# Weights mixed with float32r sums of two numbers in three products, their left-over rows on VectorE and GpSimd, and a reordered last chunk

## The chip, the cores and the metric

The kernel runs on one core of one Trainium2 chip. The metric is the device time of one execution in microseconds, given as the median of several runs.

## What is computed

Two linked computations, all in float32. First an attention through 49 "agent" rows per batch: B = 2, N = 12480 tokens, C = 128 channels. Then a two-layer network (128 to 2048 to 128, a leaky ReLU with a slope of its own for each of the 2048 features) on all 24960 tokens.

```python
a2k = sm(agents, k)            # (2, 49, 12480), softmax over the keys
agent_v = a2k @ v              # (2, 49, 128)
q2a = sm(q, agents)            # (2, 12480, 49)
x = (q2a @ agent_v).reshape(24960, 128)
h = x @ w_in                   # 128 -> 2048
g = np.maximum(h, 0.0) + alpha * np.minimum(h, 0.0)
out = g @ w_out                # 2048 -> 128
```

## The kernel before

x is never made. Since x = P · agent_v, with P the 49 softmax weights of a token, h = P · (agent_v · w_in): the kernel first makes the **mixed weights** M = agent_v · w_in (49 rows by 2048 features) of each batch, and then needs only P. P and M are each carried as two float16 numbers, a high part and what is left over, so that a product has float32's accuracy in three parts. Along the 128 rows of the contraction lie 49 rows of high parts, 49 rows again and the first 30 of 49 (`M_a`, 128 rows by 2048 columns); the remaining 19 rows with a few more (`REST` is 19, kept in groups of 32 rows, four features' tiles below one another) are `M_r`, which holds left-over parts of M.

**M before.** `mix(b, f, bank)` (L594) makes 512 columns of M in a bank of PSUM with one float32 product: `av_m`, the scaled agent values with their columns repeated in the order of the rows of `M_a`, is the stationary side, and `w_in_s[:, f*512:(f+1)*512]` is streamed. ScalarE copies the bank to float16 (`mixed_high`, L1009), VectorE puts the left-over part into rows 96 to 127 where `gate` says so (`mixed_low`, L1246). `mix_rest` (L598, its product in L602) makes the left-over rows by 16 more float32 products of 128 columns with 32 stationary columns each, four side by side in the array; `rest_high` (ScalarE, L1013) and `rest_low` (VectorE, L1251) turn these into `M_r`. `mix_linear` does the same for the linear part of the network. All this happens for batch 0 between the sums over the keys and the first chunk, and for batch 1 in the chunks of the kinds MIX (chunks 20 and 21) and MIX_REST (chunk 22).

**The chunks.** Queries go in 49 chunks: 48 of 512 tokens and a last one (number 48) of 384, half from each batch. A chunk has 8 pairs of feature tiles. For pair p, `tiles(p)` (L650, in the last chunk L647) multiplies `M_a` with the turned softmax weights `PT` into two banks, `rest_of_quad(q)` (L667, L660) adds the left-over rows for two pairs at a time with `M_r`, ScalarE makes `r_hi` (ReLU to float16, L1041), VectorE makes `r_lo` (what is left over, L1296), and `second_layer(p)` (L677) adds three products, in this order: w_hi·r_hi, w_lo·r_hi, w_hi·r_lo, each for two tiles, into the bank `OUT`. Pairs go through three slots of two banks; so `tiles(p)` waits until `r_lo` of the pair three places before it has been read out (`lo_ready`). Scores of the next chunk's queries, and of the second batch's keys in the chunks up to 10, go into the bank `SMALL` between the products of `second_layer` (L618, L868); `mix` for batch 1 uses the same bank, and the next scores wait until it has been read.

**Order around the change.** Every engine's order of work is written out by hand, engine by engine, with semaphores between them. On TensorE for batch 0: `mix(0,0)`, `mix_rest`, `mix_linear`, `tiles(0)`, `tiles(1)`, `rest_of_quad(0)`, `mix(0,1)`, `mix(0,2)`, `mix(0,3)`, and then the body of chunk 0: `second_layer(0)`, second group (`tiles(2)`, `tiles(3)`, `rest_of_quad(1)`), `second_layer(1)`, `tiles(4)`, `tiles(5)`, `rest_of_quad(2)`, `second_layer(2)` and `(3)`, `linear`, `tiles(6)`, `tiles(7)`, and so on. In MIX chunks VectorE's order is `relu_lo(3)`, `mixed_low`, `query_lo`, `relu_lo(4)`, `relu_lo(5)`; the second `mix` of the chunk lies between `second_layer(4)` and `second_layer(5)`. GpSimd has little to do: it adds the two parts of the output (`y`, L462) and copies a few columns of the stack of softmax weights (`query_again`, L443).

**The weights' place.** `w_in_s` (2048 columns, float32) is loaded by one DMA, and VectorE multiplies it by signs (L1343) for each of its four parts of 512 columns. In front of it lie the keys and behind it the values in the queue of SyncE.

## Time and profile before

| | us |
|---|---|
| runs: median (lowest to highest of 3) | 900.53 (900.29 to 901.55) |
| the profiled execution | 901.17 |
| its span from first to last instruction | 899.4 |
| TensorE matmul busy | 892.1 (99%) |
| VectorE busy | 619.2 (69%) |
| ScalarE busy | 502.4 (56%) |
| GpSimd busy | 105.5 (12%) |
| granted TensorE clock | 1.0 of full speed (2.4 GHz) |

A row of the timeline gives the start in us from the start of the span, the time from the first start to the last end of a merged group, the engine, the line, the operation, what it writes and reads by the program's names, and the number of instructions; in brackets the idle time of the engine before it and what released it. TensorE's instructions are pipelined: a group's time contains the end of the last one, so the distance between the starts of two groups is what the first costs. A float32 product is two instructions in the trace, and PEld is the weight load, which overlaps with the stream.

### The profile page before, as it was taken

The page shows a single profiled execution, that of the slowest core. Times are in us where ns is not written, and L with a number is a line of the kernel's source. Part 1 is how long each engine was busy: PE and PEld are TensorE (multiplying, and loading weights), DVE is VectorE, ACT ScalarE, POOL GpSimd, SP SyncE. Part 2 cuts the span into 40 slices and gives each one's busy share as a digit, 9 for nine tenths or more (in the row PEclk, how much of TensorE's full clock was granted, in tenths as well). Part 3 has the DMA queues.
Part 4 walks back from the last instruction along what each step waited for, and adds up shares of the span by engine and source line. Part 5 has one row for each costly group of instructions (what it writes and reads, how often), then busy time and mean ns, then how long its engine had stood idle before and what let it go on. Part 6 is the DMA issues. An engine that isn't in the chain of part 4 may idle for free.

```text
span 899.4 us, 15332 instructions
## 1 busy us (share of the span) xinstructions
PE 892.1 (99%) x5496; PEld 451.9 (50%) x5496; DVE 619.2 (69%) x883; ACT 502.4 (56%) x653; POOL 105.5 (12%) x130
## 2 busy tenths in 40 slices
PE   9999999999999999999999999999999999999998
PEld 9855555555544545444444444444444444444444
DVE  4877767766776667678666676667667676766664
ACT  2445565555555555565555566556565655665554
POOL 6500010001000100010001001011010010010100
PEclk9999999999999999999999999999999999999999
DMA  9952223122322341111112112111111121121110
GB/s 358 359 155 82 62 64 103 58 63 69 98 83 85 98 130 43 39 45 53 36 39 62 35 40 61 35 41 58 38 42 54 39 56 38 39 61 33 30 36 21
DMA packets 69975, 66.13 MB, mean 74 GB/s; under 512 B 36368, under 2 KB 54192, under 8 KB 69552
## 3 DMA queue, kind: packets, MB, share of 16 engines
q1 hardware_dynamic: 69504, 65.45, 23.9%
q8 instruction: 25, 0.41, 0.2%
q10 hardware_dynamic: 432, 0.16, 0.1%
q14 instruction: 14, 0.11, 0.0%
HBM read 41.54 MB, written 12.78 MB: 60 GB/s over the span
## 4 chain that ended last, share of the span: by engine, by line
PE 96%; DMA 2%; DVE 1%; ACT 0%; issue 0%; SPq 0%; DVEq 0%; ACTq 0%
PE ps L677 57%; PE ps L650 18%; PE ps L667 7%; PE ps L618 3%; PE ps L480 2%; PE ps L868 2%; PE ps L565 1%; PE ps L692 1%; DMA kv_s<-vP 1%; DVE r_lo L1296 1%; PE ps L595 1%; PE ps L557 1%; DMA kv_s<-kT 1%; PE ps L703 1%; PE ps L510 0%; ACT r_hi L1041 0%
## 5 line engine op out<-in xcount | busy, mean ns | idle before, releaser
L1296 DVE SCALAR_TENSOR_TENSOR r_lo<-ps,r_hi 128x1024 f16<-128x1024 f32 (+1 forms) x392 | 468.3, 1215 | 247.2 <-ACT r_hi L1041 246.8
L1041 ACT ACTIVATE r_hi<-ps 128x1024 f16<-128x1024 f32 (+1 forms) x392 | 388.6, 1017 | 261.0 <-PE ps L667 254.7
L677 PE MATMUL ps<-r_hi,w_hi 128*128 128x512 f16 (+1 forms) x784 | 244.5, 380 | 0.1
L677 PE MATMUL ps<-r_hi,w_lo 128*128 128x512 f16 (+1 forms) x784 | 241.3, 378 | 0.0
L677 PE MATMUL ps<-r_lo,w_hi 128*128 128x512 f16 (+1 forms) x784 | 234.2, 378 | 0.0
L650 PE MATMUL ps<-PT,M_a 128*128 128x512 f16 x768 | 197.6, 379 | 0.4 <-DVE r_lo L1296 0.3
L462 POOL TENSOR_TENSOR y<-y_relu,y_lin 128x512 f32<-128x512 f32 x48 | 60.7, 1266 | 599.6 <-ACT y_relu L1137 404.1
L677 PEld LDWEIGHTS ps<-r_hi,w_lo 128*128 128x128 f16 x784 | 84.5, 109 | 76.0
L677 PEld LDWEIGHTS ps<-r_lo,w_hi 128*128 128x128 f16 x784 | 78.9, 104 | 78.0
L650 PEld LDWEIGHTS ps<-PT,M_a 128*128 128x128 f16 x768 | 74.7, 98 | 81.3 <-DVE r_lo L1296 2.4
L677 PEld LDWEIGHTS ps<-r_hi,w_hi 128*128 128x128 f16 x784 | 66.7, 104 | 87.3 <-issue 40.0
L667 PE MATMUL ps<-PR,M_r 32*128 32x512 f16 x576 | 75.1, 385 | 0.0
L667 PE MATMUL ps<-PT,M_r 32*128 32x512 f16 x192 | 73.8, 384 | 0.0
L618 PEld LDWEIGHTS ps<-agents,q_s 128*128 128x128 f32 x384 | 66.6, 190 | 10.2 <-issue 0.2
L618 PE MATMUL ps<-agents,q_s 128*128 128x49 f32 x384 | 60.5, 243 | 0.0
L667 PEld LDWEIGHTS ps<-PT,M_r 32*128 32x128 f16 x192 | 17.3, 90 | 81.4 <-issue 81.0
L1033 ACT ACTIVATE stack<-q_p 128x196 f16<-128x196 f32 x49 | 18.3, 373 | 61.1 <-DVE q_p L1287 58.8
L1137 ACT ACTIVATE y_relu<-ps,out_unscale 128x512 f32<-128x512 f32 x48 | 33.0, 687 | 33.8 <-PE ps L677 33.8
L443 POOL TENSOR_TENSOR stack<-stack,ones 128x120 f16<-128x120 f16 x49 | 19.6, 400 | 163.8 <-ACT stack L1033 163.8
L1114 ACT ACTIVATE y_lin<-ps,lin_unscale 128x512 f32<-128x512 f32 x48 | 32.7, 682 | 0.0
L868 PEld LDWEIGHTS ps<-agents,kv_s 128*128 128x128 f32 x176 | 30.8, 191 | 2.6 <-DVE M_a L1246 0.4
L1161 DVE TENSOR_REDUCE k_top<-S 128x49 f32<-128x392 f32 (+2 forms) x26 | 19.9, 775 | 12.2 <-ACT S L997 12.2
(166 smaller groups left out, 491.2 us busy)
## 6 DMA issues: line engine op xcount, KB each, us to landing
q_s<-qT SPq DMA_DIRECT2D x48, 256.0 KB, 2.8
out<-y SPq DMA_DIRECT2D x48, 256.0 KB, 2.1
kv_s<-kT SPq DMA_DIRECT2D x23, 512.0 KB, 4.5
kv_s<-vP SPq DMA_DIRECT2D x12, 512.0 KB, 8.9
kv_s<-vS SPq DMA_DIRECT2D x6, 1024.0 KB, 6.1
PR<-PT SPq DMA_DIRECT2D x147, 32.0 KB, 1.9
PT<-stack SPq DMA_TRANSPOSE x196, 2.4
w_lin<-w_out SPq DMA_DIRECT2D x1, 1024.0 KB, 10.2
```

The lines of the kernel that those rows point to most:

```text
L443: pool.tensor_tensor(stack[0:T, :, 2 * A:128], stack[0:T, :, REST:A], ones[0:T, 0:4 * SPARE].rearrange("p (t a) -> p t a", a=SPARE), ALU.m ...
L462: pool.tensor_tensor(y[:, half, :], y_relu[:, half, :], y_lin[:, half, :], ALU.add).then_inc(y_ready, 1)
L618: return pe.matmul(ps[0:T, SMALL, t * A:(t + 1) * A], q_s[:, half, t * T:(t + 1) * T], agents[:, b * A:(b + 1) * A], start=True, stop=True)
L650: pe.matmul(by_tile(ps[:, 2 * slot(p) + u, 0:CHUNK]), M_a[:, b, f:f + 128], tokens(PT, half), start=True, stop=False)
L667: mm = pe.matmul(by_tile(ps[:, 2 * slot(2 * q + u // 2) + u % 2, 0:CHUNK]), M_r[32 * u:32 * u + 32, b, q * 128:(q + 1) * 128], tokens(src[ ...
L677: mm = pe.matmul(ps[:, OUT, 0:wide], w[:, 2 * p + u, :], r[:, s, u, 0:wide], start=(p == 0 and u == 0 and k == 0), stop=(p == PAIRS - 1 an ...
L868: mm = pe.matmul(ps[:, SMALL, t * A:(t + 1) * A], kv_s[:, half, t * KT:(t + 1) * KT], agents[:, A:2 * A], start=True, stop=True)
L1041: act.activation(r_hi[:, p % RING, :, 0:wide], ps[:, at:at + 2, 0:wide], ACT.Relu).then_inc(hi_ready, 1)
L1114: act.activation(y_lin[:, half, :].rearrange("p (h n) -> p h n", n=HALF), ps[:, 2 * LIN_SLOT:2 * LIN_SLOT + 2, 0:HALF], ACT.Copy, scale=li ...
L1137: act.activation(y_relu[:, half, :], ps[:, OUT, 0:CHUNK], ACT.Copy, scale=out_unscale[:, b, :]).then_inc(relu_saved, 1)
L1161: dve.tensor_reduce(k_top[:, b, m, :], by_agent(piece(b, m)), AX.X, ALU.max).then_inc(k_maxed, 1)
L1296: dve.scalar_tensor_tensor(out=r_lo[:, p % RING, :, 0:wide], in0=ps[:, at:at + 2, 0:wide], scalar=0.0, in1=r_hi[:, p % RING, :, 0:wide], o ...
```

## The change

`w_in` is split into two float32r numbers, `w_in_hi` (rounded by a ScalarE copy) and `w_in_lo` (a GpSimd subtraction), and so are the scaled agent values, `av_hi` and `av_lo` (two more VectorE steps). `mix` makes three float32r products hi·hi, hi·lo, lo·hi instead of one float32 product. `mix_rest`, `rest_high` and `rest_low` are gone: the left-over rows are taken from the same bank as `M_a`'s, by four subtractions of 19 rows by 128 columns for each `f`, written to four groups of 32 rows. VectorE does them for `f` = 0 of batch 0 and all four of batch 1 (`mixed_rest`); GpSimd does `f` = 1, 2, 3 of batch 0 (`mixed_rows`) from a float32 copy in SBUF that ScalarE makes (`mixed_out`), together with the work of `mixed_low` for them. For batch 0 the second `mix` is moved to the place of `mix_rest`. `w_in` is loaded in two DMAs into `y_lin` and `y_relu`, `w_inT` into `r_lo`, which are free until the first chunk. In the last three chunks the first two products of `second_layer(4)` go before `tiles(7)`, and in the last chunk `second_layer(7)` begins with its four products of `r_hi` before `r_lo` is there. `M_r` is cleared by GpSimd at the start.

```diff
             def mix(b, f, bank):
-                pe.matmul(ps[:, bank, :], av_m[:, b, 0:128], w_in_s[:, f * 512:(f + 1) * 512], start=True,
-                          stop=True).then_inc(m_raw, 1)
-
-
-            def mix_rest(b, bank):
-                for t in range(FT):
-                    q, g = t // 4, t % 4 * 32
-                    mm = pe.matmul(ps[g:g + 32, bank, q * 128:(q + 1) * 128], av_m[:, b, 128:SEL],
-                                   w_in_s[:, t * 128:(t + 1) * 128], start=True, stop=True, skip_group_check=True)
-                mm.then_inc(r_raw, 1)
+                pe.wait_ge(win_lo, f + 1)
+                at = slice(f * 512, (f + 1) * 512)
+                pe.matmul(ps[:, bank, :], av_hi[:, b, :], w_in_hi[:, at], start=True, stop=False)
+                pe.matmul(ps[:, bank, :], av_hi[:, b, :], w_in_lo[:, at], start=False, stop=False)
+                pe.matmul(ps[:, bank, :], av_lo[:, b, :], w_in_hi[:, at], start=False, stop=True).then_inc(m_raw, 1)
...
             pe.wait_ge(b_av, 1)
             mix(0, 0, F_BANK[0])
-            mix_rest(0, REST_BANK[0])
+
+            pe.wait_ge(b_rows, 2)
+            mix(0, 1, F_BANK[1])
             mix_linear(0, LIN_BANK[0])

             pe.wait_ge(k_saved, FULL + 1 + EARLY)
-            pe.wait_ge(m_low, 1)
+            pe.wait_ge(m_first, 1)
             pe.wait_ge(q_turned, 64)
             tiles(0, 0, 0)
             tiles(1, 0, 0)
-            pe.wait_ge(r_low, 1)
+            pe.wait_ge(r_first, 1)
             pe.wait_ge(q_spread, 48)
             rest_of_quad(0, 0, 0)
-            mix(0, 1, F_BANK[1])
-            pe.wait_ge(l_low, 1)
+
             mix(0, 2, F_BANK[2])
...
                     if start:
 
-                        second_layer(0, half, wide)
-                        pe.wait_ge(m_low, 3)
+                        second_layer(0, half, wide, None, (0, 1))
+                        pe.wait_ge(lo_ready, 1)
+                        second_layer(0, half, wide, None, (2,))
+
+                        pe.wait_ge(m_out, 2)
+                        pe.wait_ge(l_low, 1)
+
+                        pe.wait_ge(m_low, 1)
+                        pe.wait_ge(r_low, 1)
                         second_group()
...
                     pe.wait_ge(lo_ready, g + 2)
+                    if start:
+
+                        pe.wait_ge(m_low, 2)
+                        pe.wait_ge(r_low, 2)
                     tiles(4, half, b)
...
                         elif kind == MIX:
-                            pe.wait_ge(m_low, 5 + 2 * half)
+                            pe.wait_ge(m_second, 1 + 2 * half)
+                            pe.wait_ge(r_second, 1 + 2 * half)
...
+                    if start:
+
+                        pe.wait_ge(m_low, 3)
+                        pe.wait_ge(r_low, 3)
                     tiles(6, half, b)
+
+                    early = 0 if there(n + 3) else 1
+                    second_layer(4, half, wide, None, range(0, early))
                     pe.wait_ge(lo_ready, g + 6)
                     tiles(7, half, b)
                     rest_of_quad(3, half, b)
                     rest_of_linear(half, b)
-                    second_layer(4, half, wide)
+                    second_layer(4, half, wide, None, range(early, 3))
...
                     second_layer(6, half, wide)
-                    pe.wait_ge(lo_ready, g + 8)
-                    second_layer(7, half, wide)
+                    if there(n + 1):
+                        pe.wait_ge(lo_ready, g + 8)
+                        second_layer(7, half, wide)
+                    else:
+
+                        pe.wait_ge(hi_ready, g + 8)
+                        second_layer(7, half, wide, None, (0, 1))
+                        pe.wait_ge(lo_ready, g + 8)
+                        second_layer(7, half, wide, None, (2,))
```

On GpSimd (before `query_again(1)`, and the new rows after it) and on ScalarE and VectorE:

```diff
+            for f in range(FT // 4):
+                at = slice(f * 512, (f + 1) * 512)
+                pool.wait_ge(win_hi, f + 1)
+                pool.tensor_tensor(w_in_lo[:, at], w_in_bank(f), w_in_hi[:, at], ALU.subtract).then_inc(win_lo, 1)
             query_again(1)
+            def mixed_rows(f):
+                pool.wait_ge(m_high, f + 1)
+                pool.wait_ge(m_out, f)
+                m = M_a[96:128, 0, f * 512:(f + 1) * 512]
+                then(pool.tensor_scalar(m, m, gate[96:128, :], None, ALU.mult))
+                pool.tensor_tensor(m, m, mixed_s[96:128, f % 2, :], ALU.add).then_inc(m_low, 1)
+                pool.wait_ge(m_low, f)
+                for u in range(4):
+                    at = f * 512 + u * 128
+                    mr = pool.tensor_tensor(M_r[32 * u:32 * u + REST, 0, f * 128:(f + 1) * 128],
+                                            mixed_s[0:REST, f % 2, u * 128:(u + 1) * 128], M_a[0:REST, 0, at:at + 128],
+                                            ALU.subtract)
+                    if u < 3:
+                        then(mr)
+                mr.then_inc(r_low, 1)
+                pool.wait_ge(r_low, f)
...
             mixed_high(0, 0, F_BANK[0])
-            rest_high(0, REST_BANK[0])
+            mixed_high(0, 1, F_BANK[1])
+            mixed_out(1, F_BANK[1])
             linear_high(0)
             relu_hi(0, 0, 0, True)
-            mixed_high(0, 1, F_BANK[1])
+            relu_hi(1, 0, 1, True)
             mixed_high(0, 2, F_BANK[2])
-            relu_hi(1, 0, 1, True)
+            mixed_out(2, F_BANK[2])
             mixed_high(0, 3, F_BANK[3])
+            mixed_out(3, F_BANK[3])
...
+                then(dve.tensor_scalar(av_m[:, :], av_raw[:, 0:128], m_scale[:, b, 0:1], M_SCALE, ALU.mult, ALU.mult))
+                then(dve.tensor_copy(av_hi[:, b, :], av_m[:, :]))
+                dve.tensor_tensor(av_lo[:, b, :], av_m[:, :], av_hi[:, b, :], ALU.subtract).then_inc(b_av, 1)
...
+            def mixed_rest(b, f, bank):
+                dve.wait_ge(r_clear, 1)
+                dve.wait_ge(m_high, FT // 4 * b + f + 1)
+                for u in range(4):
+                    at = f * 512 + u * 128
+                    mr = dve.tensor_tensor(M_r[32 * u:32 * u + REST, b, f * 128:(f + 1) * 128],
+                                           ps[0:REST, bank, u * 128:(u + 1) * 128], M_a[0:REST, b, at:at + 128], ALU.subtract)
+                mr.then_inc((r_first, r_second)[b], 1)
```

## Rows read from the trace of the kernel before

**Rows 1.** The page: span and busy time by engine.

```profile
span 899.4 us, 15332 instructions
PE 892.1 (99%) x5496; PEld 451.9 (50%) x5496; DVE 619.2 (69%) x883; ACT 502.4 (56%) x653; POOL 105.5 (12%) x130
```

**Rows 2.** Busy time by stretch: length, PE, PEld, DVE, ACT, POOL, clock, DMA.

```profile
46.00:50.00 4.00, 3.21 (x49) 2.51 (x49) 1.68 (x3) 0.00 (x0) 0.00 (x0) 1.00 1.01 263
...
54.70:58.60 3.90, 3.90 (x51) 2.00 (x50) 2.85 (x8) 1.62 (x4) 0.00 (x0) 1.00 0.76 249
```

**Rows 3.** Timeline of TensorE, the mixing for batch 0 and chunk 0.

```profile
54.70 1.09 PE L595 MATMUL ps<-w_in_s,av_m 128*128 128x512 f32 x2
55.72 1.08 PE L602 MATMUL ps<-w_in_s,av_m 128*32 128x128 f32 x32
...
58.59 2.84 PE L595 MATMUL ps<-w_in_s,av_m 128*128 128x512 f32 x6
61.27 0.59 PE L677 MATMUL ps<-r_hi,w_hi 128*128 128x512 f16 x2
...
62.57 1.03 PE L650 MATMUL ps<-PT,M_a 128*128 128x512 f16 x4
...
65.93 1.03 PE L650 MATMUL ps<-PT,M_a 128*128 128x512 f16 x4
```

**Rows 4.** Timeline of VectorE and ScalarE in the same stretch.

```profile
54.04 0.30 DVE L1236 TENSOR_SCALAR av_m<-av_raw,m_scale 128x160 f32<-128x160 f32 x1
...
55.82 0.60 ACT L1009 ACTIVATE M_a<-ps 128x512 f16<-128x512 f32 x1 [1.28 <-PE ps L595]
...
56.45 0.76 DVE L1246 SCALAR_TENSOR_TENSOR M_a<-M_a,gate,ps 32x512 f16<-32x512 f16 x1 [0.53 <-ACT M_a L1009]
...
58.71 1.02 ACT L1041 ACTIVATE r_hi<-ps 128x1024 f16<-128x1024 f32 x1 [0.82 <-PE ps L667]
```

**Rows 5.** Groups by line, of GpSimd and VectorE: busy us, mean ns, idle before.

```profile
L462 POOL TENSOR_TENSOR y<-y_relu,y_lin 128x512 f32<-128x512 f32 x48 | 60.7, 1266 | 599.6 <-ACT y_relu L1137 404.1 <-issue 195.6
L443 POOL TENSOR_TENSOR stack<-stack,ones 128x120 f16<-128x120 f16 x49 | 19.6, 400 | 163.8 <-ACT stack L1033 163.8
L422 POOL TENSOR_SCALAR sigma<-sigma 128x16 f32<-128x16 f32 x1 | 0.3, 283 | 0.1
...
L1257 DVE TENSOR_TENSOR L_b<-ps,L_rh 64x128 f16<-64x128 f32 x2 | 0.6, 282 | 0.0
```

**Rows 6.** Timeline of VectorE, one operation beside GpSimd's work and without it.

```profile
36.65 0.86 DVE L1287 TENSOR_TENSOR q_p<-q_e,q_rec 128x196 f32<-128x196 f32 x1
...
45.33 0.36 DVE L1287 TENSOR_TENSOR q_p<-q_e,q_rec 128x196 f32<-128x196 f32 x1
```

**Rows 7.** Timeline of TensorE and VectorE in chunk 20 (MIX) and chunk 22.

```profile
424.22 0.76 DVE L1246 SCALAR_TENSOR_TENSOR M_a<-M_a,gate,ps 32x512 f16<-32x512 f16 x1
...
425.58 2.35 DVE L1296 SCALAR_TENSOR_TENSOR r_lo<-ps,r_hi 128x1024 f16<-128x1024 f32 x2 [0.22 <-ACT r_hi L1041]
...
427.85 1.03 PE L650 MATMUL ps<-PT,M_a 128*128 128x512 f16 x4
...
456.16 1.08 PE L602 MATMUL ps<-w_in_s,av_m 128*32 128x128 f32 x32
457.18 0.61 PE L677 MATMUL ps<-r_hi,w_hi 128*128 128x512 f16 x2
```

**Rows 8.** Timeline of chunks 47 and 48, the last two.

```profile
876.44 0.59 PE L650 MATMUL ps<-PT,M_a 128*128 128x512 f16 x2
877.21 0.60 PE L650 MATMUL ps<-PT,M_a 128*128 128x512 f16 x2 [0.18 <-DVE r_lo L1296]
...
894.02 0.49 PE L677 MATMUL ps<-r_hi,w_hi 128*128 128x384 f16 x2
...
894.27 0.96 DVE L1296 SCALAR_TENSOR_TENSOR r_lo<-ps,r_hi 128x768 f16<-128x768 f32 x1 [0.37 <-ACT r_hi L1041]
895.29 0.50 PE L677 MATMUL ps<-r_hi,w_hi 128*128 128x384 f16 x2
```

More of the change, by code:

```diff
@@ L112, in build @@
         av_abs = sb("av_abs", [C, A])
-        av_m = sb("av_m", [C, B, SEL])
+        av_m = sb("av_m", [C, 128])
+        av_hi = sb("av_hi", [C, B, 128], F32R)
+        av_lo = sb("av_lo", [C, B, 128], F32R)
         av_l = sb("av_l", [C, B, SEL])
@@ L1412, in body @@
                         mixed_low(1, 2 * half, SMALL)
[L1413 to L1414 removed]
+                        mixed_rest(1, 2 * half, SMALL)
                     if there(n + 2):
```

92 lines of the change are left out of this document (50 added, 42 removed).

## The prediction

> **What bounds the kernel now.** I read the page first: TensorE is busy 99% of the span, and no other engine above 69% [rows 1]. Then the busy time by stretch, to find where TensorE is not full. From 46 to 50 us it is busy 3.21 us of 4.00 with a DMA share of 1.01: the transfers of the values set the pace there [rows 2], so nothing that only moves work of ScalarE, VectorE or GpSimd before 50 us can cost or gain. From 54.7 us on it is full (3.90 of 3.90) [rows 2]. From there on a TensorE instruction that goes is worth its time, and an operation added elsewhere costs nothing until TensorE waits for it. So three places decide: the mixing for batch 0 with chunk 0, the MIX chunks, and the end. Last I read the timeline of these.
>
> **Batch 0: what goes.** The two float32 instructions of the first mix start at 54.70; the next group starts at 55.72. Six instructions (three mixes) start at 58.59 and last 2.84 us [rows 3], of which the last instruction's own tail is about 0.2, so a mix is (2.84 - 0.2)/3 = 0.87 us, or 0.43 for one of its two instructions. No row shows a float32r product. Bounds: as cheap as float16's 512 columns, whose pairs cost (1.03 - 0.16)/4 = 0.22 us each within a group of four [rows 3]; as dear as a whole float32 product, 0.87. I take 0.22, because a float32 instruction of 0.43 is just two streams of 0.22 (so a float32 product is four streams), and I assume that an operand of float32r, having no second part, is streamed once. A mix is then 3 x 0.22 = 0.65, 0.21 less. The trade stops paying at 0.87/3 = 0.29 us a product.
> The Trainium skill (FP8 and Floating Point Precision, TensorE Precision Notes) says the same of float32, four passes, and that the reduced form truncates to 22 bits on reading; by one pass a product the sum stays as it is.
> mix_rest costs 1.02 us in chunk 22, from 456.16 to the start of second_layer at 457.18 [rows 7], and about as much at 55.72.
>
> **Batch 0: what comes instead.** I follow each engine.
> (a) VectorE now makes av_m, av_hi and av_lo in a dependent row. av_m starts at 54.04 and takes 0.30 [rows 4]; two more steps at 0.3 bring b_av to about 54.95, so TensorE starts at 55.05 in place of 54.70: +0.35. Three products end at 55.70, where two float32 instructions ended at 55.55. ScalarE's M_a copy comes 0.27 after the end of the stream (55.82 [rows 4]), now at 55.95; VectorE's 0.76 [rows 4] follow, so tiles(0) starts near 57.4, as before plus 0.1.
> (b) The second mix ends at 56.35. ScalarE: M_a copy to 57.2, the new mixed_out(1), at the 0.60 of the M_a copy [rows 4], to 57.8. linear_high after it is behind nothing that TensorE waits for soon.
> (c) GpSimd's mixed_rows. Its prices: two-input operations of 512 columns 1.27 us and of 120 columns 0.40; a one-input operation of 16 columns 0.28 [rows 5]. The gate multiplication has one input and 512 columns: between 0.28 and 1.27, I take 0.7. The addition: 1.27. Four subtractions of 128 columns: 4 x 0.42 = 1.7. Each waits for the one before, some 0.09 each, 0.5 together. One f is 4.2 us (3.4 to 5.0).
> For the gate multiplication, the Trainium skill (GPSIMD Engine Reference, Engine selection) calls one-input operations "roughly line-rate" and two-input ones about twice as slow as VectorE; by it the estimate is at most 0.65, where I take 0.7 from between the rows.
> So f = 1 is ready at 57.9 + 4.2 = 62.1, f = 2 at 66.4, f = 3 at 70.7.
> (d) TensorE: tiles(0) to rest_of_quad(0) until 58.75, two mixes until 60.05. second_layer(0) has r_hi then (ScalarE's 1.02 us from about 58.9, cf. 58.71 [rows 4]); its last part waits for r_lo until 61.2 and ends at 61.65. The second group waits for bank 4: ScalarE has relu_hi(0), relu_hi(1), the M_a copy and mixed_out(2) in a row from 58.9, 2 x 1.02 + 2 x 0.60, until 62.15. GpSimd's f = 1 comes at 62.1. So the second group starts at 62.25, where it was 62.57 [rows 3]: the TensorE time saved so far has nearly all turned into waiting. second_layer(1) with its scores ends 3.36 us later (65.93 - 62.57 [rows 3]), at 65.6, and there tiles(4) waits for f = 2 until 66.5. It was 65.93: **+0.6**. The f = 3 rows (70.7) are early for tiles(6), some 5.3 us after tiles(4). With 3.4 us an f it would be -0.3, with 5.0 (f = 2 at 67.9) +2.0.
> (e) VectorE beside a busy GpSimd: the same multiplication takes 0.86 us there and 0.36 alone [rows 6]. GpSimd's four subtractions for w_in_lo (4 x 1.27, from about 46.1) end near 51.3, where the scaling of the selection (0.3 us, on the way to av_m) may be held some 0.1. In chunk 0 query_sum and query_norm may be held 1 us, which the 0.6 above covers. **+0.1** (0 to 0.5).
> The skill (GPSIMD Engine Reference, Key points) names contention for VectorE instructions with two SBUF inputs or in a 2-port mode. The 0.86 agrees; relu_lo, with one input in PSUM, should stay as it is.
> Under cover: ScalarE's four roundings of w_in (2.4 us) lie in its wait from 45.5 to 50.1, behind the DMA-bound stretch [rows 2]; the clear of M_r is at GpSimd's idle start; query_again(2) queues behind mixed_rows until 71, and its transposes have their old time at lin_ready, near 73. If that cover went, chunk 2 would wait.
>
> **Batch 1 (MIX).** VectorE gets mixed_rest behind mixed_low: four subtractions of 128 columns from PSUM. The nearest row is 0.28 for that very shape in 64 rows [rows 5]; back to back some of it overlaps, so 0.95 for four (0.6 to 1.15). In chunk 20, mixed_low starts at 424.22 and the next two relu_lo at 425.58 after 0.22 idle, ending at 427.93 [rows 7]. They now end at 427.93 + 0.95 - 0.22 = 428.66. tiles(7) starts 0.43 behind tiles(6), at 428.28 [rows 7], and waits for them: 428.71, +0.43, whatever TensorE saved before. (The wait for r_second before the scores falls into the same loss.) The second mix of the chunk saves its 0.21; its mixed_rest fits into 1.3 us of VectorE's idle time. Two chunks: 2 x (0.43 - 0.21) = **+0.4** (-0.8 without the stall, +0.9).
> MIX_REST: mix_rest gone, nothing in its place, **-1.0**.
>
> **End.** In chunk 47, tiles(6) starts at 876.44 and its two products are over at 876.87; tiles(7) starts at 877.21, released by r_lo [rows 8]. That 0.34 is filled with 0.43 of second_layer(4): -0.34, and the same in chunk 46. In chunk 48 the same gap is filled, but r_lo(6) sets what follows, so nothing is gained there. second_layer(7) starts at 895.29, when r_lo is done (894.27 + 0.96) [rows 8]. second_layer(6) started at 894.02 with 0.98 of products, so the four early ones run from 895.0 to 895.65 and the last two to 895.98 instead of 896.27: -0.3. **-1.0** (-0.3 to -1.1).
>
> **Sum:** +0.6 + 0.1 + 0.4 - 1.0 - 1.0 = -0.9, against the profiled execution's 901.17 (span 899.4 and 1.8 around it), so 900.3. That execution was 0.6 above the median of 900.53. For the median: **899.7 us**. Ends together: -3.3 (897.2) and, with the dear ends of (c), (e) and MIX, +2.2 (902.7).
>
> **Rivals.**
> 1. *No new waits.* GpSimd needs 3.4 us an f or less and VectorE's four subtractions hide. Then each mix's 0.21 counts: start -0.3, MIX -0.85, rest -1.0, end -1.1: 897.3. For it: VectorE is only 69% busy. Against it: VectorE has just 0.22 us of idle time before relu_lo(4) [rows 7]. Halfway cases, one of two stalls gone, reach 898.5.
> 2. *GpSimd is the new bound.* If its step takes 5.5 us, by contention or by slow dispatch of small operations in 32 rows, f = 2 ends at 68.9 and tiles(4) is 3 us late: 899.7 + 2.4 = 902.1. It decides from 3.9 us an f, from which tiles(4) is late at all.
> 3. *float32r isn't cheap.* At 0.43 a product (both halves of a float32 instruction) a mix is 1.29, 0.43 more than before; MIX +1.7, the start about +2.2 since both mixes are ahead of GpSimd's rows, with the -2.0 of rest and end: 902.5, slower. At 0.87 a product: a mix 2.6, MIX +6.8, start +4.5: about 910. It decides from 0.29 us. For it: float32 products pay double per instruction. Against it: the operands have no second part to stream.
> 4. *The end's order does nothing*, because r_lo comes later by as much: 900.7.
>
> **How the numbers follow.** Forecast with rival 4 and the small shifts: 0.66. Rival 1 and its halfway cases: 0.22. Rival 2: 0.05. Rival 3: 0.07. About 0.2% (1.8 us) is what a measurement of this kernel can tell from no change. Below 898.7: rival 1's better part and the low edge of the forecast, 0.22. Above 902.3: rival 3, part of rival 2, and the forecast's edge, 0.12. Within: 0.66. The range takes in the ends of the sum, 897.1 to 902.7, and leaves out the dear case of rival 3.
>
> **What would show it.** L650 of pair 4 near 66.5 with a wait for a GpSimd line before it, mixed_rows of f = 2 ending there; the second group near 62.25; float32r products 0.22 apart; in chunks 20 and 21 a gap of 0.4 us of TensorE ahead of tiles(7) or second_layer(3), released by VectorE; 1.0 us less in chunk 22; no gap after tiles(6) in chunks 46 and 47, and the last product 0.3 us after r_lo plus two products. It is wrong if float32r products are more than 0.29 apart, if GpSimd's step is far from 4.2 us, or if something before 50 us moves the whole.

## The result and the profile after

| | before | after |
|---|---|---|
| median of 7 runs (lowest to highest), us | 900.78 (900.29 to 902.0) | 904.24 (902.34 to 904.74) |
| profiled execution, us | 901.17 | 904.19 |
| span, us | 899.4 | 902.5 |
| mean granted TensorE clock of the span | 1.0 | 0.996 |

The kernel is slower: the ratio is 1.0038, with a 95% interval of 1.0029 to 1.0046. The forecast was 899.7 us and no change that can be measured; the time lies above the upper end of the range, 902.7. In 6 of the 7 runs of the kernel after the mean clock was below 1.0; the seventh, at 1.0, took 902.34 us.

The page of the kernel after, first its busy times, then the clock in 40 slices:

```profile
span 902.5 us, 15292 instructions
PE 892.6 (99%) x5440; PEld 454.2 (50%) x5440; DVE 625.6 (69%) x902; ACT 505.0 (56%) x658; POOL 125.7 (14%) x153
...
PEclk9989999999999999999999999999999999999999
```

TensorE has 56 instructions fewer and yet is busy 892.6 us, where it was 892.1 [rows 1]. One slice of the clock (45 to 68 us) shows an 8. The shares say no more, so I compared positions: in each chunk the addition of y on GpSimd starts at a time that can be read in both traces, and the difference between the kernels tells where the time went.

| chunk | start before, us | after against before, us |
|---|---|---|
| 0 | 80.18 | +4.14 |
| 19 | 419.31 | +4.14 |
| 20 (MIX) | 437.61 | +4.61 |
| 21 (MIX) | 455.90 | +5.09 |
| 22 (MIX_REST) | 474.16 | +4.07 |
| 45 | 853.25 | +4.07 |
| 46 | 869.47 | +3.72 |
| 47 | 885.43 | +3.37 |
| end of the span | 899.4 | +3.1 |

All that is lost is lost ahead of chunk 0's end, and a little in the two MIX chunks; chunks 1 to 19 and 23 to 45 are untouched. The busy times by stretch of the kernel after (length, PE, PEld, DVE, ACT, POOL, clock, DMA share, GB/s) show the kind of the loss, beside [rows 2]:

```profile
50.00:54.70 4.70, 3.35 (x24) 3.08 (x24) 3.72 (x11) 0.72 (x3) 2.38 (x3) 0.90 0.26 66
54.70:58.60 3.90, 3.90 (x13) 3.07 (x13) 2.16 (x9) 0.99 (x2) 0.00 (x0) 0.50 0.70 235
58.60:62.50 3.90, 3.90 (x19) 2.00 (x19) 2.19 (x7) 2.31 (x5) 2.22 (x2) 0.74 0.37 109
62.50:66.00 3.50, 2.98 (x14) 1.02 (x12) 2.35 (x2) 3.21 (x6) 3.08 (x6) 1.00 0.12 27
```

Two different things are seen. From 50 to 54.7 and from 62.5 us TensorE waits (3.35 of 4.70, 2.98 of 3.50). From 54.7 to 58.6 it is full, as before, but at a granted clock of 0.50, that is 1.2 GHz, and it gets through 13 instructions where it got through 51 [rows 2] (the counts do not compare as they stand, since 32 of the 51 are the short products of mix_rest; the times of equal groups, below, do). The timeline of the kernel after names the parts:

```profile
53.16 0.39 PE L642 MATMUL ps<-av_abs,ones 128*128 128x49 f32 x2 [1.22 <-DVE av_abs L1306]
54.35 1.83 PE L664 MATMUL ps<-agents,q_s 128*128 128x49 f32 x8
55.97 0.77 PE L648 MATMUL ps<-w_in_hi,av_hi 128*128 128x512 f32 x1
56.54 0.63 PE L649 MATMUL ps<-w_in_lo,av_hi 128*128 128x512 f32 x1
56.97 0.63 PE L650 MATMUL ps<-w_in_hi,av_lo 128*128 128x512 f32 x1
...
61.92 0.39 PE L649 MATMUL ps<-w_in_lo,av_hi 128*128 128x512 f32 x1
62.16 0.40 PE L650 MATMUL ps<-w_in_hi,av_lo 128*128 128x512 f32 x1
62.39 0.39 PE L648 MATMUL ps<-w_in_hi,av_hi 128*128 128x512 f32 x1
65.17 1.02 PE L696 MATMUL ps<-PT,M_a 128*128 128x512 f16 x4 [0.52 <-POOL M_r L493]
70.08 1.02 PE L696 MATMUL ps<-PT,M_a 128*128 128x512 f16 x4 [1.54 <-POOL M_r L493]
```

The same comparison can be made free of the transfers, whose timing differs between executions: the last 16 instructions of the value sums start at 48.96 us before and at 48.18 after (call it V). From V, tiles(4) starts at 65.93 - 48.96 = 16.97 before and at 70.08 - 48.18 = 21.90 after: 4.93 us later, where the prediction had 0.7. From V the first mix starts at 5.74 before and 7.79 after.

On VectorE and GpSimd of the kernel after:

```profile
45.45 4.11 DVE L1351 SCALAR_TENSOR_TENSOR w_lo<-w_relu,w_scale,w_hi 128x512 f16<-128x512 f32 x3
50.77 1.76 DVE L1351 SCALAR_TENSOR_TENSOR w_lo<-w_relu,w_scale,w_hi 128x512 f16<-128x512 f32 x1
...
48.98 3.01 POOL L479 TENSOR_TENSOR w_in_lo<-y_relu,w_in_hi 128x512 fp32r<-128x512 f32 x2
60.20 1.57 POOL L488 TENSOR_SCALAR M_a<-M_a,gate 32x512 f16<-32x512 f16 x1 [6.31 <-ACT mixed_s L1089]
61.85 1.17 POOL L489 TENSOR_TENSOR M_a<-M_a,mixed_s 32x512 f16<-32x512 f16 x1
63.10 1.92 POOL L493 TENSOR_TENSOR M_r<-mixed_s,M_a 19x128 f16<-19x128 f32 x4
```

The fourth w_lo (weights_low) took 0.74 us before and takes 1.76 here: it begins at 50.77 and ends at 52.53, 0.54 behind the end of GpSimd's last subtraction for w_in_lo (51.99). The value read and its absolute value stand behind it on VectorE, and TensorE waits 1.22 us for av_abs. And one step of mixed_rows is 1.57 + 1.17 + 1.92 and the gaps, 4.9 us.

### The profile page after: what moved, and what is told of

The parts are those of the page before. It is cut to its first block, busy times and chain, and to the rows that moved or that the text cites. A ratio compares the mean times of both kernels' runs of the same rounds, so it can differ in the third digit from the quotient of the medians.

```text
span 902.5 us, 15292 instructions
## 1 busy us (share of the span) xinstructions
PE 892.6 (99%) x5440; PEld 454.2 (50%) x5440; DVE 625.6 (69%) x902; ACT 505.0 (56%) x658; POOL 125.7 (14%) x153
## 4 chain that ended last, share of the span: by engine, by line
PE 96%; DVE 2%; DMA 1%; ACT 1%; POOL 1%; issue 0%; DVEq 0%; POOLq 0%
PE ps L725 57%; PE ps L696 18%; PE ps L713 7%; PE ps L664 3%; PE ps L531 3%; PE ps L915 1%; PE ps L616 1%; PE ps L740 1%; DMA kv_s<-vP 1%; DVE r_lo L1384 1%; PE ps L608 1%; PE ps L751 1%; ACT r_hi L1117 1%; PE ps L758 0%; PE ps L561 0%; PE ps L693 0%
```

## The experiments

Theory A was, after reading this trace: three losses at the start add up, a held w_lo that stops TensorE, a clock that falls after that, and GpSimd's step that is too long; and in MIX, VectorE's mixed_rest. Rival B: the three float32r products, or the work as such, let the clock fall, whether TensorE has waited or not. Rival C: GpSimd holds VectorE whatever stands where, and moving one operation only moves the loss to another.

**The held w_lo taken out of the row.**

```diff
             selection_scaled(0, K_BANK)
-            weights_low(3)
             values_out(0, W_BANK)
             values_scaled(0, K_BANK)
+            weights_low(3)
```

> The changed kernel with one VectorE operation moved: the fourth left-over of the second layer's weights (w_lo, two inputs in SBUF) goes behind the scaling of the agent values instead of ahead of them. In the changed kernel it took 1.76 us beside GpSimd's subtraction (0.74 before), TensorE then stood idle for 1.2 us, and its granted clock was 0.50 in the stretch 54.7 to 58.6 us. Theory A (held VectorE operation, idle TensorE, clock falls): the idle shrinks to under 0.5 us, the clock stays at 1.00, the first float32r product starts near 54.9 instead of 55.97, the products are 0.23 apart instead of 0.43; GpSimd's rows then start 2.3 us earlier and the whole is 2 to 2.5 us faster, about 901.8 us. Rival B (the clock falls because of the float32r products or the longer row of av_m, av_hi, av_lo): products still 0.43 apart, gain at most 0.8 us, about 903.5. Rival C (another operation is held in its place): the idle stays over 1 us, 904.

Measured: 902.13 us (901.1 to 904.76, 10 runs), 1.0021 of before (1.0012 to 1.0031). The profiled execution has the clock at 1.0 throughout. TensorE in it:

```profile
52.61 0.39 PE L642 MATMUL ps<-av_abs,ones 128*128 128x49 f32 x2 [0.34 <-DVE av_abs L1306]
54.67 0.51 PE L648 MATMUL ps<-w_in_hi,av_hi 128*128 128x512 f32 x1
62.63 1.02 PE L696 MATMUL ps<-PT,M_a 128*128 128x512 f16 x4 [0.58 <-POOL M_r L493]
67.53 1.02 PE L696 MATMUL ps<-PT,M_a 128*128 128x512 f16 x4 [1.53 <-POOL M_r L493]
```

The wait ahead of av_abs is 0.34 in place of 1.22, the scores take their usual time, and tiles(4) is 19.04 from V: 2.86 less than in the kernel after, 2.07 more than before. The waits for GpSimd are what they were, 0.58 and 1.53. Rival B falls: the same three products run at the full clock. The trace of the kernel after says the same: in stretches of 1 us its mean clock is 0.90 from 53 to 54 us and 0.50 from 54 on, and av_m (54.30) and the first float32r product (55.97) come behind that. In 2 of 10 runs the mean clock was 0.996 all the same (904.76 and 903.64 us; the others 901.1 to 902.56), so the fall isn't gone, it has become rare. No trace was kept of these two.

**Work for TensorE ahead of the wait.**

```diff
             pe.wait_ge(b_dened, 1)
+            warm(4)
             value_sums(0, K_BANK)
```

> The changed kernel with four more float32 products of 128 columns (about 1.0 us, their result unused) where TensorE stood idle ahead of the sums of the agent values; everything else as it is, so VectorE's held operation stays. Theory A: the clock stays at 1.00, the float32r products are 0.23 apart, the first starts near 55.3 (VectorE's lateness stays), about 902.1 us. Rival D (the lateness is the cost, the clock costs little): 903.9 or more, because only pacing changes. Rival B (float32r products lower the clock by themselves): products 0.43 apart, 904.2.

Measured: 902.77 us (902.05 to 903.06, 10 runs), 1.0021 (1.0012 to 1.0031), with the clock at 1.0 in all 10 runs. tiles(4) is 19.95 from V. Here GpSimd held another operation of VectorE, the scaling of the selection, and TensorE waited for that:

```profile
52.11 0.51 PE L638 MATMUL ps<-rec_sel,av_rows 128*128 128x160 f32 x2 [0.88 <-DVE rec_sel L1293]
```

The four products went in behind this wait, from 52.87 us on, and the wait ahead of av_abs was gone. So the clock was kept though an operation was held and TensorE waited for it. The clock and the held operation are two losses, and each can be removed without the other. What the trace alone does not tell apart is the products and the wait itself, which was shorter in this execution (0.88 us in place of 1.22); for the products speak the 10 runs, none with the clock fallen. At 902.77 us the time lies between theory A (902.1) and rival D (903.9), and the products were 0.23 apart, against rival B.

**The end's order alone, on the kernel before.**

```diff
-            def second_layer(p, half, wide, after=None):
+            def second_layer(p, half, wide, after=None, parts=(0, 1, 2)):
...
                     tiles(6, half, b)
+                    early = 0 if there(n + 3) else 1
+                    second_layer(4, half, wide, None, range(0, early))
                     pe.wait_ge(lo_ready, g + 6)
...
-                    second_layer(4, half, wide)
+                    second_layer(4, half, wide, None, range(early, 3))
...
+                        pe.wait_ge(hi_ready, g + 8)
+                        second_layer(7, half, wide, None, (0, 1))
+                        pe.wait_ge(lo_ready, g + 8)
+                        second_layer(7, half, wide, None, (2,))
```

> The kernel before with only the end's order changed (the first two products of second_layer(4) ahead of tiles(7) in the last three chunks, second_layer(7) begun with r_hi). Theory: 0.35 us less in chunk 46, 0.35 in chunk 47, 0.27 at the end, in all 1.0 us faster than before, about 899.8. Rival: the gain belongs to the changed alignment after the slower start, and alone it is 0.3 or less.

Measured: 899.2 us (898.8 to 899.73, 10 runs), 0.9987 (0.9977 to 0.9997). The same kernel went once more in a later job, beside the kernels at the end of this section:

> The kernel before with only the end's order changed, once more on the chip of the version for batch 1 alone, to compare the two: 1.0 to 1.3 us faster than before, and 1.5 us slower than that version.

It took 899.31 us (898.67 to 899.86, 11 runs), 0.9988 (0.9979 to 0.9997). In both traces chunks 46 and 47 are 0.35 us shorter each. This part of the change is a gain and nothing else.

**Batch 1's rows from VectorE to GpSimd.** ScalarE copies the mix out (second_out), and GpSimd subtracts in the same chunk, where it is idle:

```diff
+            def second_rows(f):
+                pool.wait_ge(m_high, FT // 4 + f + 1)
+                pool.wait_ge(m_out, 4 + f)
+                for u in range(4):
+                    at = f * 512 + u * 128
+                    mr = pool.tensor_tensor(M_r[32 * u:32 * u + REST, 1, f * 128:(f + 1) * 128],
+                                            mixed_s[0:REST, f % 2, u * 128:(u + 1) * 128], M_a[0:REST, 1, at:at + 128],
+                                            ALU.subtract)
...
                         mixed_low(1, 2 * half, SMALL)
-                        mixed_rest(1, 2 * half, SMALL)
```

> The changed kernel with batch 1's left-over rows made by GpSimd from a float32 copy of ScalarE (as batch 0's are), instead of VectorE's four subtractions of 1.17 us. Theory: TensorE's wait of 0.58 us ahead of second_layer(3) in chunks 20 and 21 goes, and the two chunks cost 0.6 us less each: 1.2 us faster than the changed kernel, about 903.0. Rival: ScalarE's copy of 0.6 us pushes r_hi(4) and r_lo back by as much, and the wait only moves to tiles(7): 904.

Measured: 903.1 us (901.63 to 903.96, 8 runs), 1.0028 (1.0017 to 1.0039). Over chunks 20, 21 and 22 the change against before is -0.18, -0.26 and -1.11 us, where the kernel after had +0.47, +0.48 and -1.02: 1.48 us less. The rows of the kernel after in chunk 20 show what is gone, VectorE first:

```profile
429.15 1.17 DVE L1337 TENSOR_TENSOR M_r<-ps,M_a 19x128 f16<-19x128 f32 x4
430.46 0.38 PE L725 MATMUL ps<-r_hi,w_hi 128*128 128x512 f16 x1 [0.58 <-DVE M_r L1337]
```

Four subtractions take 1.17 us, 0.29 each, and do not overlap; TensorE waits 0.58 for them before second_layer(3). With GpSimd doing them (1.92 us for four, beside other work) there is no such wait, and the rival expectation, 904, did not come. The start of this execution was worse (chunk 0 at +5.21), for a reason that the next line shows:

```profile
50.92 1.32 DVE L1317 TENSOR_SCALAR rec_sel<-sel,rec_col 128x160 f32<-128x160 f32 x1
```

The edit touches nothing there, and yet it was rec_sel that was held (0.30 in the kernel after) and not w_lo, which took 0.74. In the kernel after rec_sel starts at 50.55, 0.1 us ahead of GpSimd's last subtraction; here it starts at 50.92, just behind it (50.88), and ends at 52.24, 0.10 behind that instruction's end. Which of VectorE's operations meets GpSimd's instruction is thus decided by tenths of a microsecond, which differ between executions. In 6 of the 8 runs the mean clock was 0.996 (902.86 to 903.96 us), in 2 it was 1.0 (901.63 and 901.69).

**GpSimd busy in the kernel before.** This kernel has no float32r at all. GpSimd makes four subtractions whose result nobody uses; everything that the kernel computes stays.

```diff
             query_again(0)
+            pool.wait_ge(whi_ready, 1)
+            for f in range(4):
+                pool.wait_ge(w_signed, f + 1)
+                then(pool.tensor_tensor(y_relu[:, f % 2, :], w_in_s[:, f * 512:(f + 1) * 512],
+                                        w_in_s[:, f * 512:(f + 1) * 512], ALU.subtract))
             query_again(1)
```

> The kernel before with four subtractions of 128 by 512 float32 on GpSimd from the end of ScalarE's w_hi on (their result is used by nothing), as the changed kernel has them; nothing else changed, float32 products as before. Theory A (VectorE's operations with two inputs in SBUF or in a two-port form are held by GpSimd, TensorE idles, the clock falls): an operation of the chain rec_sel, w_lo, av_raw, av_abs takes 0.6 to 1.1 us longer, TensorE idles about 1 us more, in most executions the granted clock falls to 0.50 for some us; 1 us slower where it does not fall and 2.5 to 3 us slower where it does, median 903. Rival B (the changed kernel's start is late through its longer row of scalings and its float32r products): same as before, 900.6.

Measured: 901.29 us (900.8 to 901.78, 10 runs), 1.0008 (0.9999 to 1.0017). GpSimd, VectorE and TensorE in it:

```profile
46.25 5.38 POOL L456 TENSOR_TENSOR y_relu<-w_in_s 128x512 f32<-128x512 f32 x4 [2.18 <-ACT w_hi L1027]
46.21 4.53 DVE L1268 SCALAR_TENSOR_TENSOR w_lo<-w_relu,w_scale,w_hi 128x512 f16<-128x512 f32 x3
50.94 0.35 PE L583 MATMUL ps<-den_col,pairs 128*128 128x1 f32 x2 [1.35 <-DVE den_col L1365]
54.70:58.60 3.90, 3.90 (x51) 2.43 (x50) 2.90 (x9) 2.00 (x5) 0.00 (x0) 1.00 0.85 299
```

The three w_lo took 4.53 us, where they took 2.07 before. That made den_col late and TensorE wait 1.35 us for it. Chunk 0 is at +0.54 while V was 0.97 earlier, so the hold cost 1.5 us in this execution: GpSimd's subtractions alone, without float32r, are enough to hold VectorE and make TensorE wait. The medians are 0.83 us apart, and the interval still takes in no change, so for the whole kernel the loss is not clear of the noise. Theory A had the hold right, but not its place (it named rec_sel to av_abs) and not its size (903). The last line, of this kernel's stretches, shows what theory A doesn't explain: after an idle time as long as the kernel after's, the clock stayed at 1.0, here and in all 10 runs.

**The roundings of w_in earlier**, so that GpSimd's subtractions end before the value read:

```diff
                 if m == 9:
                     query_exp(1)
+                if 7 <= m < 11:
+                    f = m - 7
+                    at = slice(f * 512, (f + 1) * 512)
+                    act.wait_ge(w_signed, f + 1)
+                    act.activation(w_in_hi[:, at], w_in_bank(f), ACT.Copy).then_inc(win_hi, 1)
             weights_high()
-            for f in range(FT // 4):
-                at = slice(f * 512, (f + 1) * 512)
-                act.wait_ge(w_signed, f + 1)
-                act.activation(w_in_hi[:, at], w_in_bank(f), ACT.Copy).then_inc(win_hi, 1)
```

> The changed kernel with ScalarE's four roundings of w_in between the exponentials of the keys 7 to 10 instead of behind w_hi, so that GpSimd can begin its subtractions at 43.4 us and is done before the sums over the values are (49 us). Theory A: no VectorE operation after 49 us is held, the clock stays at 1.00, the first float32r product starts 6.2 us after the last group of the value sums instead of 7.8, and the whole is as with the moved w_lo, 901.8 to 902.2 us, with less spread. Rival C: the held operations of w_lo move into the critical stretch, 903.5.

Measured: 903.95 us (902.09 to 906.47, 6 runs), 1.0034 (1.0021 to 1.0046). VectorE and TensorE of the profiled execution, and one of its stretches:

```profile
45.77 1.27 DVE L1370 TENSOR_SCALAR q_den<-q_sum 128x4 f32<-128x4 f32 x1
47.28 1.17 DVE L1376 TENSOR_TENSOR q_p<-q_e,q_rec 128x196 f32<-128x196 f32 x1
48.38 3.08 DVE L1352 SCALAR_TENSOR_TENSOR w_lo<-w_relu,w_scale,w_hi 128x512 f16<-128x512 f32 x3
51.66 0.38 PE L629 MATMUL ps<-den_col,pairs 128*128 128x1 f32 x2 [1.30 <-DVE den_col L1449]
54.70:58.60 3.90, 3.90 (x18) 3.81 (x18) 1.93 (x10) 0.50 (x1) 0.00 (x0) 0.50 0.62 192
```

In this execution the expectation failed. The first three w_lo started at 48.38, where they started at 45.45 in the kernel after. The row ahead of them on VectorE began 1.2 us later, and GpSimd, now busy earlier, held two of its operations: q_den (1.27 us, 0.17 in the kernel after) and q_p (1.17, there 0.36). weights_high had ended by 47.01 and was not what they waited for. They ran into the time of den_col, and TensorE waited 1.30 us again. The clock fell (mean 0.994) in 3 of 6 runs (905.36 to 906.47 us; the others 902.09 to 902.54). In the traced execution rival C was right: the loss only moved. The three runs at the full clock took nearly what theory A had, 901.8 to 902.2.

**w_lo moved, and GpSimd left with the subtractions alone.** On top of the first experiment VectorE makes mixed_low for all of batch 0, as before, and the gate multiplication and the addition go from GpSimd. ScalarE's relu_hi(1) also goes back behind the copies of f = 2.

```diff
             def mixed_rows(f):
                 pool.wait_ge(m_high, f + 1)
                 pool.wait_ge(m_out, f)
-                m = M_a[96:128, 0, f * 512:(f + 1) * 512]
-                then(pool.tensor_scalar(m, m, gate[96:128, :], None, ALU.mult))
-                pool.tensor_tensor(m, m, mixed_s[96:128, f % 2, :], ALU.add).then_inc(m_low, 1)
-                pool.wait_ge(m_low, f)
...
             mixed_rest(0, 0, F_BANK[0])
+            mixed_low(0, 1, F_BANK[1])
             linear_low(0)
             relu_lo(0, 0)
+            mixed_low(0, 2, F_BANK[2])
             relu_lo(1, 1)
+            mixed_low(0, 3, F_BANK[3])
```

> The kernel with the moved w_lo, and besides VectorE makes the rows 96 to 127 of M_a for f = 1, 2, 3 of batch 0 as it did before (0.76 us each), so that GpSimd has only its four subtractions of 19 rows an f. In the changed kernel GpSimd's one-input multiplication takes 1.57 us, its addition 1.17 and the four subtractions 1.92, 4.9 us an f with the gaps. Theory E (GpSimd's pace of 4.9 us an f sets tiles(4) and the second group): the waits of 0.58 and 1.53 us for GpSimd go, 2.0 us faster than with the moved w_lo alone, 900.1 us. Rival F (ScalarE's four copies and two ReLUs in a row, or VectorE, are late next): 0.8 us or less of it is gained, 901.3 or more.

Measured: 900.71 us (899.43 to 903.02, 10 runs), 1.0004 (0.9995 to 1.0013). TensorE's two waits for GpSimd are gone:

```profile
63.64 1.02 PE L692 MATMUL ps<-PT,M_a 128*128 128x512 f16 x4 [0.38 <-DVE M_a L1325]
66.92 1.06 PE L692 MATMUL ps<-PT,M_a 128*128 128x512 f16 x4
```

tiles(4) is 17.78 from V, 1.26 less than with w_lo moved alone, though rec_sel was held in this execution (1.03 us in place of 0.30). From the first mix to tiles(4) it is 11.03 us, where it was 12.86 with w_lo moved alone and 11.23 before. The median is 1.4 us below that of w_lo moved alone, between theory E's 2.0 and rival F's 0.8: a wait of 0.38 for VectorE's mixed_low has come in. The clock fell in 2 of 10 runs (902.95 and 903.02).

**All four edits together** (the roundings earlier, w_lo later, mixed_low on VectorE, batch 1's rows on GpSimd):

> All together: early roundings of w_in, w_lo moved, rows 96 to 127 on VectorE for batch 0, left-over rows of batch 1 on GpSimd. Theory: 902.0 (first two) - 2.0 (GpSimd's pace) - 1.3 (MIX chunks) = 898.7 us, 1.8 us faster than the kernel before and 0.5 us faster than the kernel before with the end's order alone (899.2). Rival: the waits move to ScalarE's copies, 900 or more.

Measured: 898.92 us (898.25 to 902.98, 12 runs), 0.9987 (0.9978 to 0.9995). tiles(4) is 17.19 from V, 0.22 behind before; chunks 20 to 22 give 1.54, and the end its 1.0. One of 12 runs had the clock fallen (902.98). The theory had 898.7. The early roundings, beside a held q_den (0.96) and q_p (1.18), made den_col only 0.14 us later than before here.

**Batch 0 as before, batch 1 and the end changed.** Batch 0 keeps its float32 mix. w_in is split during chunks 8 to 11, where ScalarE and GpSimd have time, and only batch 1 uses float32r and the rows on GpSimd (w_inT lies in r_lo, as in the kernel after):

```diff
+                    if isinstance(n, int) and 8 <= n < 12:
+                        f = n - 8
+                        at = slice(f * 512, (f + 1) * 512)
+                        act.wait_ge(w_signed, f + 1)
+                        act.activation(w_in_hi[:, at], w_in_s[:, at], ACT.Copy).then_inc(win_hi, 1)
...
+                if b == 1:
+                    pe.wait_ge(win_lo, f + 1)
+                    at = slice(f * 512, (f + 1) * 512)
+                    pe.matmul(ps[:, bank, :], av_hi[:, :], w_in_hi[:, at], start=True, stop=False)
+                    pe.matmul(ps[:, bank, :], av_hi[:, :], w_in_lo[:, at], start=False, stop=False)
+                    pe.matmul(ps[:, bank, :], av_lo[:, :], w_in_hi[:, at], start=False, stop=True).then_inc(m_raw, 1)
```

> The kernel before with the end's order, and with float32r products for batch 1 alone: batch 0 is mixed as before, w_in is rounded by ScalarE and its left-over made by GpSimd in chunks 8 to 11 (GpSimd idle there, behind lin_saved, where VectorE reads PSUM), and batch 1's left-over rows come from a float32 copy of ScalarE by GpSimd, so that mix_rest goes. Theory (all losses of the change are in the start, its gains in the MIX chunks and at the end): against the end's order alone (899.2) 1.1 us less for mix_rest in chunk 22 and 0.2 us less in each of the MIX chunks, about 897.8 us, with the granted clock at 1.00 in all executions and a start as before. Rival: the roundings and subtractions in chunks 8 to 11 hold TensorE as much as they save, 899.2 or more.

Measured: 897.94 us (897.62 to 898.7, 10 runs), 0.9975 (0.9965 to 0.9984), with the clock at 1.0 in every run. Chunks 20 to 22 give 1.48 us and the end 1.0; the roundings in chunks 8 to 11 cost at most 0.06. It is the fastest of all, and beats both kernels: the idea is a gain where the engines that help have time, and a loss where they haven't. Beside it, in the same job, the end's order alone took 899.31, so float32r and the rows on GpSimd for batch 1 are worth 1.4 us.

## Why the prediction was wrong

**What bounds the kernel, and "before 50 us nothing can cost": in part wrong.** ScalarE's four roundings and GpSimd's start did lie behind the transfers, and the three w_lo that grew from 2.07 to 4.11 us cost only 0.14 in the kernel after (den_col's product starts 1.59 from V, before 1.45). But the cover ends with the value sums, and GpSimd's subtractions go on until 51.99, where the prediction had 51.3, since each took 1.3 to 1.7 us and not 1.27. With the roundings earlier (3.08 us, starting later), and with GpSimd busy in the kernel before (4.53), the three w_lo reached TensorE through den_col.

**(a) and (b): right, a little dear.** With w_lo moved the first mix is 6.18 from V, before 5.74, so 0.44 later. Of that 0.17 lies ahead of den_col (1.62 from V, before 1.45), which the three held w_lo delay; the dependent row of av_m, av_hi and av_lo, from av_abs to the first mix, is 2.06 in place of 1.80. It cost 0.26, against 0.35. GpSimd starts its rows 2.99 behind the first mix, where (b) had 2.85.

**The float32r product: right.** In the start the products are 0.24 and 0.23 us apart (61.92, 62.16, 62.39), and 0.43 apart at the clock of 0.50 (56.54, 56.97). Rival 3 is refuted. A detail: behind rest_of_quad the first product of a mix costs more, as the rows of chunk 20 show:

```profile
423.71 0.50 PE L648 MATMUL ps<-w_in_hi,av_hi 128*128 128x512 f32 x1
424.05 0.39 PE L649 MATMUL ps<-w_in_lo,av_hi 128*128 128x512 f32 x1
424.28 0.40 PE L650 MATMUL ps<-w_in_hi,av_lo 128*128 128x512 f32 x1
424.52 0.60 PE L725 MATMUL ps<-r_hi,w_hi 128*128 128x512 f16 x2
```

It is 0.34 to the second product here, and the mix is 0.81 in all; at this place it took 0.96 before. The mix later in the chunk is recorded as starting before the group ahead of it has run out, so it is read from the starts around it: from the last group of second_layer(4) to second_layer(5) it is 1.13 us (434.87 to 436.00), before 1.29 (430.11 to 431.40), of which 0.43 is that group. So this mix takes 0.70 in place of 0.86. Each mix saves 0.15 or 0.16, not 0.21.

The Trainium skill (FP8 and Floating Point Precision, TensorE Precision Notes) has float32 as four passes and the reduced form as reading truncated operands; the 0.23 us per product beside 0.87 for a float32 one agrees with one pass against four.

**(c) and (d), GpSimd's step: mis-sized, and rival 2 in part right.** I had 4.2 us with an upper end of 5.0; it is 4.9. The gate multiplication, taken at 0.7 between 0.28 and 1.27, is 1.57, above its upper bound; the addition is 1.17 (1.27), the four subtractions 1.92 (1.7), with less between the steps. The prediction's own working gives +1.8 for 4.9 us (f = 2 ready at 57.9 + 9.8 = 67.7, against 65.93), and with w_lo moved the part from the first mix to tiles(4) grew by 12.86 - 11.23 = 1.63, where the prediction had 66.5 - 55.05 = 11.45, or 0.22 more than before: 1.4 of the miss. With GpSimd left the subtractions alone that part was 11.03. Rival 2 had 0.05, and needed 5.5 us for its 2.4; the mechanism had a larger chance than that, since the step of 3.9 us from which it costs was below my own estimate. Rival 1, no new waits, is refuted by the waits of 0.52 and 1.54 us for GpSimd.

The Trainium skill (GPSIMD Engine Reference, Engine selection) calls one-input operations roughly line-rate. This trace disagrees: 1.57 us for 512 columns in 32 partitions with the gate as a scalar operand, where two inputs of the same shape took 1.17. The measurement decides. Whether the scalar from memory, the place (in and out are the same) or the type makes it dear was not tried.

**(e), VectorE beside GpSimd: the step that failed first.** I priced it at 0.1 (0 to 0.5), for the scaling of the selection. That operation is one of those that can be held, but the price was a small growth. In the traces where rec_sel was held, it did not grow by a factor: it ended 0.10 us behind the end of GpSimd's instruction, whatever was left of it, and these instructions took 1.3 to 1.7 us each. w_lo, the very next one, is as exposed; by the rows of before it began at 51.41, just behind the 51.3 at which I had GpSimd done, but in this execution the values came 0.78 us earlier and GpSimd ended at 51.99. From the product with rec_sel to that with av_abs it is 2.16 us, before 1.26: the held w_lo cost 0.90 us of TensorE's time, and the three w_lo ahead of den_col 0.14. rec_sel, when it was the one held, took 1.03 and 1.32 in place of 0.30. relu_lo, with an input in PSUM, stayed as it was (1.22 us), as I had said.

The rule of the Trainium skill (GPSIMD Engine Reference, Key points), contention for VectorE instructions with two inputs in SBUF or in a 2-port mode, agrees with w_lo, which has two such inputs, and with relu_lo, which was not held. rec_sel and q_den have one tensor in SBUF as input and were held, so by the rule they ran in a 2-port mode; no trace shows an operation's mode.

**Not foreseen: the clock.** The prediction has no term for it and names it nowhere. Behind the wait from 51.9 to 53.2 us the granted clock fell to 0.50 (between 53 and 54 us) and came back between 60 and 61. From the product with av_abs to the first mix it is 2.81 us, with w_lo moved 2.06: 0.75 for the clock. The part from the first mix to tiles(4) is 14.11 - 12.86 = 1.25 longer than with w_lo moved, with the same work. That is 2.0 us together. Taken step by step, from before to w_lo moved and from there to the kernel after, the terms are 0.14 (the three w_lo) + 0.90 (the held w_lo) + 0.26 (the row) + 0.75 (the clock, up to the first mix) + 1.63 (GpSimd) + 1.25 (the clock, behind it) = 4.93, the measured one. Without the clock's fall the time would have been about 904.2 - 2.0 = 902.2 us, an estimate, and in the range, as the run at 902.34 us was, though (c) and (e) would have been as wrong: the width of the range, and not the working, would have covered them.

**MIX: the mechanism right, the size off.** A stall released by VectorE was predicted, at tiles(7) or second_layer(3), worth +0.22 net a chunk. It is at second_layer(3), with 0.58 us of idle time. By the starts it costs 0.75 us (429.28 to 430.46, of which 0.43 is work), where the prediction had 0.43 and took the wait for r_second to fall into the same loss. Less two mixes' saving of 0.15 and 0.16 that is 0.44, nearly all of the +0.47 and +0.48 that a chunk is longer. Mis-sized are mixed_rest, 1.17 in place of 0.95 (I let the four overlap, and they don't), the wait for it, and the mix's own saving.

**MIX_REST and the end: right.** -1.02 for -1.0 in chunk 22. Chunks 46 and 47: -0.35 each, for -0.34; the last one -0.27, for -0.3. Rival 4 is refuted by the experiment as well. The rows of the last products of the kernel after stand 0.32 to 0.33 apart right to the end, no wait for r_lo among them:

```profile
898.65 0.49 PE L725 MATMUL ps<-r_hi,w_lo 128*128 128x384 f16 x2
898.97 0.49 PE L725 MATMUL ps<-r_lo,w_hi 128*128 128x384 f16 x2
```

**In sum.** Three steps failed in the start, beside the wait in MIX: (e), the held VectorE operations, were priced at 0.1 and cost 1.04; (c), GpSimd's step, was taken at 4.2 us and is 4.9, which cost 1.4 at tiles(4); and the clock had no term and cost 2.0. So 0.7 predicted for the start became 4.93 from V, or 4.14 in these two executions, whose transfers differ by 0.78 in V; +0.4 in MIX became +0.95; the two gains came as told. 4.14 + 0.95 - 1.02 - 0.35 - 0.35 - 0.27 = 3.10, the 3.1 of the spans.

**What stays open.** Why the clock fell in 6 of the 7 runs of the kernel after, in 3 of 6 with the roundings earlier and in 6 of 8 with batch 1's rows moved, but in none of the 10 with GpSimd busy in the kernel before, where TensorE was idle as long (1.35 us). From 50 to 54.7 us TensorE is busy 3.30 of 4.70 us in the latter, in the profiled execution, and 3.35 in the kernel after, so the busy share does not tell them apart. With w_lo moved the fall was rare (2 of 10), and with a few products ahead of the value sums there was none in 10. That a wait is part of the cause is argued from this, not shown, and what is added to it is not known. The traces give no length of wait that decides it: the clock stayed up behind 1.35 us there and fell behind 1.14, 1.22 and 1.30 us in the three traces in which it fell.

## What to carry to other kernels

Before work is given to an idle engine, look which instructions of its neighbours it can hold. Give the range of the forecast room for a hold of up to the whole length of the instruction that holds, on any operation of the dependent row in the stretch, and do not price it at a mean growth. A price for an operation on GpSimd that no row shows should be bounded above the dearest similar row, since one input was no cheaper than two here. And of a change with several parts, read each part's position in the trace: here the end and batch 1's mixing are worth 2.5 us together once they stand alone, in a change that as a whole made the kernel 3.5 us slower.

## What the runs showed of the hardware

- A fall of the TensorE clock to 1.2 GHz around 55 us cost the kernel after 2.0 us in its trace. The medians of the runs of one kernel with the clock at 1.0 and of those with it fallen are 902.34 and 904.25 (after), 901.66 and 903.38 (batch 1's rows moved), 901.8 and 904.2 (w_lo moved), 900.2 and 903.0 (w_lo moved, subtractions alone), 902.3 and 905.5 (the roundings earlier), 898.9 and 903.0 (all four edits): 1.7 to 4.1 us apart. Part of that can be a longer hold in the same runs, since few of them were traced.
- A VectorE operation held by GpSimd: 0.30 became 1.03 and 1.32 us (rec_sel, 128x160, one SBUF input), 0.17 became 1.27 (q_den, 128x4, one SBUF input), 0.74 became 1.76 (w_lo, 128x512, two SBUF inputs); an operation from PSUM was untouched (r_lo, 1.22). In turn GpSimd's four 128x512 subtractions took 1.32 to 1.71 us each beside VectorE's w_lo, where its addition of the same size takes 1.27 on its own [rows 5].
- A float32r product of 512 columns follows the one before it after 0.23 us at the full clock and 0.43 at half of it; the first behind rest_of_quad takes 0.34.
- A GpSimd operation is hardly cheaper for fewer partitions: four of 19x128 took 1.92 us, 0.48 each, where 128x120 takes 0.40 [rows 5], and an addition of 32x512 took 1.17 where 128x512 takes 1.27 [rows 5] (the types differ in both pairs).
- Four VectorE subtractions of 19x128 from PSUM, one behind the other, took 1.17 us, 0.29 each.
